# Another order for the last router unit, the z unit and the second expert tile between two phases of a fused kernel

## The reference, cut to what matters

```python
xread, sread = attention both ways between x [4,8,512,64] and state [4,8,32,64]
x = concat([xread, sread], axis=2)  -> 2176 tokens of 512      # 4 x (512 + 32)
h = x @ w_in                                                  # 512 -> 2048
x = (h * tanh(softplus(h))) @ w_out                           # 2048 -> 512
logits = cosine(x, expert_emb) / tau                          # 8 experts
e = argmax(logits); gate = softmax(logits)[e]
out = gate * (relu(x @ w1[e]) @ w2[e])                        # 512 -> 1024 -> 512
```

## Time and profile before

| what | us |
|---|---|
| median of three runs (lowest, highest) | 701.31 (697.56, 705.27) |
| the profiled execution | 701.31 |
| its span, first to last instruction | 699.5 |
| PE busy in it | 657.1 |
| DVE busy, ACT busy, POOL busy | 442.5, 385.9, 50.8 |

### The profile page before, as it was taken

How to read it: one execution, slowest core, us unless ns; L and a number is a source line. 1 busy time by engine, 2 the same in 40 slices (tenths; PEclk the granted TensorE clock), 3 DMA queues, 4 the chain that set the end, 5 groups by cost and what they waited for, 6 DMA issues and landing times.

```text
span 699.5 us, 12384 instructions
## 1 busy us (share of the span) xinstructions
PE 657.1 (94%) x4142; PEld 513.4 (73%) x4143; DVE 442.5 (63%) x687; ACT 385.9 (55%) x501; POOL 50.8 (7%) x75
## 2 busy tenths in 40 slices
PE   7889979999989999899999999889999999999995
PEld 5667657687767787676578877678888888888883
DVE  6899889979548699685677658462722452262261
ACT  2789678785547887477787453252622442261250
POOL 1000000000200002000000103001001010010101
PEclk9999999999989999999999999999999999999998
DMA  9713453000814000344000531472621360153140
GB/s 264 218 32 107 151 166 121 0 2 2 269 45 135 37 2 31 95 137 154 9 1 8 219 106 77 162 261 76 220 82 45 109 211 30 45 197 134 45 150 5
DMA packets 35350, 72.72 MB, mean 104 GB/s; under 512 B 5699, under 2 KB 5699, under 8 KB 35312
## 3 DMA queue, kind: packets, MB, share of 16 engines
q1 hardware_dynamic: 27728, 56.93, 25.3%
q0 software_dynamic: 3040, 9.13, 3.3%
q10 hardware_dynamic: 4544, 6.14, 2.9%
HBM read 60.92 MB, written 12.16 MB: 104 GB/s over the span
## 4 chain that ended last, share of the span: by engine, by line
PE 64%; DVE 16%; ACT 10%; issue 5%; DMA 4%; SPq 0%; ACTq 0%; POOL 0%; DVEq 0%; POOLq 0%
PE PS L708 16%; PE PS L736 16%; PE PS L613 11%; PE PS L569 7%; DVE ww L1384 3%; PE PS L717 3%; PE PS L524 3%; DMA raw<-in_w 2%; PE PS L478 2%; ACT ww L981 2%; DVE qq L1396 2%; ACT rr L977 2%; DVE qq L1379 2%; DVE gl L1402 2%; ACT rr L975 1%
## 5 line engine op out<-in xcount | busy, mean ns | idle before, releaser
L613 PE MATMUL PS<-WH,gh 128*128 128x512 f32 x256 | 103.3, 404 | 0.8 <-DVE gl L1402 0.8
L613 PE MATMUL PS<-WH,gl 128*128 128x512 f32 x256 | 101.0, 395 | 0.0
L613 PE MATMUL PS<-WL,gh 128*128 128x512 f32 x256 | 101.0, 394 | 0.0
L1067 ACT ACTIVATE hh<-PS 128x512 fp32r<-128x512 f32 x42 | 23.0, 596 | 96.4 <-PE PS L717 94.3
L736 PE MATMUL PS<-WH,hh 128*128 (+1 forms) x168 | 68.6, 409 | 3.1 <-DVE hl L1488 2.0
L1478 DVE TENSOR_TENSOR WL<-raw,WH 128x1024 f32 (+1 forms) x48 | 56.2, 1222 | 23.5 <-ACT WH L1047 23.4
L736 PE MATMUL PS<-WH,hl 128*128 (+1 forms) x168 | 66.5, 396 | 0.0
L736 PE MATMUL PS<-WL,hh 128*128 (+1 forms) x168 | 66.2, 394 | 0.0
L1379 DVE SCALAR_TENSOR_TENSOR qq<-ww,PS 128x1024 f32<-128x1024 f32 (+1 forms) x35 | 41.5, 1187 | 35.5 <-ACT ww L965 35.4
L981 ACT ACTIVATE ww<-ww,cst 128x1024 f32<-128x1024 f32 (+1 forms) x35 | 39.4, 1127 | 41.6 <-DVE ww L1384 41.6
L613 PEld LDWEIGHTS PS<-WH,gh 128*128 128x128 f32 x256 | 48.2, 188 | 18.8 <-issue 7.5
(11 more groups left out here) (252 smaller groups left out, 1281.8 us busy)
## 6 DMA issues: line engine op xcount, KB each, us to landing
raw<-in_w SPq DMA_DIRECT2D x48, 512.0 KB, 4.6
raw<-in_w_in SPq DMA_DIRECT2D x36, 512.0 KB, 4.9
yg<-by_expert ACTq DMA_DIRECT2D x22, 260.0 KB, 3.4
raw<-in_w_out SPq DMA_DIRECT2D x8, 512.0 KB, 4.6
by_expert<-junk SPq DMA_DIRECT2D x1, 2080.0 KB, 10.2
wr<-in_w_in SPq DMA_DIRECT2D x4, 512.0 KB, 9.4
x_0a<-in_x SPq DMA_DIRECT2D x8, 128.0 KB, 3.0
x_0b<-in_x SPq DMA_DIRECT2D x8, 128.0 KB, 3.6
```

Of the source, the lines that this page charges most:

```text
L613: mm = pe.matmul(PS[:, 2 + t, :], a[:, v % 2, e, t * P:t * P + P], w[:, 8 + p, e * 512:e * 512 + 512], start=(p == 0 and e == 0 and i == 0 ...
L1067: a.activation(hh[:, 4 * j:4 * j + 4, :], PS[:, 3 + j, :].rearrange("p (k m) -> p k m", k=4), ACT.Copy).then_inc(hh_rdy, 1)
```

## The change

`GT(3)` goes from behind step 31 to behind the first half of `YB(2)`, after the loop; `TY(t0)` goes ahead of the whole of `Y(31)`. The four transposed tiles of unit 3 use the banks 6, 3, 4, 6 in place of 3, 4, 5, 6: tile 0 waits for bank 6 to be free, and tile 3 for the copy of tile 0. `route_k(3)` goes ahead of `YB(3)`, `route_k("z")` ahead of `PB(t0)`, `TY(t1)` behind half of `PB(t0)`. On ACT `split_gz(3)` goes ahead of `y_hi(t0)`, `load(t1)` from ahead of `y_out(3)` to behind `relu(t0, 1)`, with a new wait for all scatters of unit 3; two squares go ahead of the two `turned(3, ...)`; `load(t2)` goes ahead of `h_hi(t1, 1)`. On DVE `lo_gz(3)` goes ahead of `y_lo(t0)` and `second_tile` behind `route_b(3)`. On POOL `scatter(3)` goes ahead of `root("z")`.

```diff
         def t_bank(c, t):
-            return (3, 4, 5, 6)[t] if c == 3 else 6
+            return (6, 3, 4, 6)[t] if c == 3 else 6
...
             root(3)
+            scatter(3)
             root("z")
-            scatter(3)
             scatter("z")
...
-                if c == 3 and t == 3:
+                if c == 3 and t == 0:
                     pe.wait_ge(gz_lo, 4)
+                elif c == 3 and t == 3:
+                    pe.wait_ge(rt_e, 3 * ST + 1)
...
-                if second(t):
-                    pe.wait_ge(idx_rdy, RU[3] + 1)
...
                     if p == 7:
-                        Y(v, (0,))
                         TY(t0)
-                Y(v, (1,) if v == 0 or v == B * PC - 1 else (0, 1))
+                Y(v, (1,) if v == 0 else (0, 1))
...
                     if p == 7:
-                        GT(3)
                         YB(2, (0, 1))
+            GT(3)
             for t in range(ST):
                 route_t(3, t)
             for t in range(ST):
                 route_l(3, t)
             YB(2, (2, 3))
+            route_k(3)
             YB(3)
-            route_k(3)
             PA(t0, (0,))
             route_t("z", 0)
             PA(t0, (1,))
-            t1 = (0, 1)
             TR(t0, (0,))
             route_l("z", 0)
             TR(t0, (1,))
+            route_k("z")
+            PB(t0, (0, 1, 2, 3))
+            t1 = (0, 1)
             TY(t1)
-            PB(t0, (0, 1))
-            route_k("z")
-            PB(t0, (2, 3))
             PB(t0, (4, 5))
             PA(t1)
...
                     act.wait_ge(e1_rdy, 1)
+                    act.wait_ge(scattered, 16 * 4 * ST)
...
             whi(0, 2, 0)
+            split_gz(3)
             y_hi(t0)
             whi(0, 3, 0)
+            y_out(3)
+            squares(3, (0, 1))
+            turned(3, 0)
+            turned(3, 2)
+            squares(3, (2, 3))
+            gate_exp(3)
+            y_out("z")
+            whi(0, 4, 0)
+            squares("z", (0,))
+            whi(0, 5, 0)
             t1, t2 = (0, 1), (0, 2)
-            load(t1)
-            y_out(3)
-            split_gz(3)
-            turned(3, 0)
-            squares(3, (0,))
-            turned(3, 2)
-            squares(3, (1, 2, 3))
-            whi(0, 4, 0)
-            gate_exp(3)
-            whi(0, 5, 0)
-            y_out("z")
-            squares("z", (0,))
-            whi(0, 6, 0)
             relu(t0, 0)
             turned("z", 0)
+            whi(0, 6, 0)
+            relu(t0, 1)
+            load(t1)
             whi(0, 7, 0)
-            relu(t0, 1)
             h_hi(t0, 0)
             h_hi(t0, 1)
             gate_exp("z")
...
             h_hi(t1, 0)
-            h_hi(t1, 1)
             act.wait_ge(tab_rdy, 3)
             less4 = act.value_load(etab[0:1, E_LESS4:E_LESS4 + 1], min_val=NT - 4, max_val=WT - 4)
             load(t2)
+            h_hi(t1, 1)
...
             wlo(0, 2, 0)
+            lo_gz(3)
             y_lo(t0)
             wlo(0, 3, 0)
-            second_tile()
             y_out(3)
-            lo_gz(3)
             turned(3, 1)
             turned(3, 3)
             route_a(3)
             route_b(3)
+            second_tile()
+            y_out("z")
             wlo(0, 4, 0)
             wlo(0, 5, 0)
-            y_out("z")
             wlo(0, 6, 0)
```

## The result

| | kernel before | kernel after |
|---|---|---|
| median us (lowest, highest, executions) | 700.92 (697.56, 705.27, 4) | 709.66 (705.73, 714.18, 4) |
| ratio, 95% interval | | 1.0137 [1.0101, 1.0172] |
| profiled execution, its span | 701.31, 699.5 | 706.29, 704.5 |
| mean granted clock of the profiled execution | 0.983 | 0.986 |

What follows compares the result with a forecast made beforehand. PE was taken as the bound, busy 657.1 of 699.5 us. Landing t2 4.5 us later plus 3.4 us of half clock gave +7.9: span 707.4, with 1.8 around it 709.2 us; range 703.0 to 714.0.

Steps and rivals of the forecast that it cites:

- 4.5 of waits: Between Y(31) and t2's landing: the landing comes at 449.6 in place of 445.1 us at full clock, +4.5 us.
- 3.4 of half clock: One half-clock fall at the stall ahead of route_t(3), one at that ahead of PB(t0), 1.7 us each.
- The hand-over: To unit 3's router: split_gz(3), ahead of y_out(3), waits for GT(3), so route_t(3) starts at 410.3, 3.0 us later.
- `route_k(3)` early earns: route_k(3) ahead of YB(3): 12 matmuls (2.8 us) leave the path; row numbers at 420.5, winning back all 3.9 us lost.
- The second tile: t1's DMA waits for unit 3's scatters, holding PB(t0) until 432.7; y_lo(t1) starts 6.0 us later, at 437.0.
- `load(t2)` first: load(t2) ahead of h_hi(t1,1): issued 0.95 us behind the table, landing 12.6 behind y_lo(t1) in place of 14.1, gaining 1.5.
- The clock: TensorE's half-clock falls on the new path: 3.4 us taken, from bounds of none (0) to 6.6.
- Rival (b): Half clock holds through the router, three falls in a row plus one: 4.5 + 6.6 = +11.1, 712.4 us; chance 0.19.
- Rival (a): Stalls come but the clock holds, or falls only under work off the path: +4.5, 705.8 us; chance 0.30.
- Rival (c): y_out(3), freed from load(t1), starts right behind Y(31), route_t(3) 2.3 us earlier: -3.8, 697.5 us; chance 0.05.

Runs made afterwards that it cites:

- e1: Kernel after with split_gz(3) and lo_gz(3) again behind y_out(3) and tile banks 3, 4, 5, 6: 706.68 us, ratio to before 1.0120.
- e12: Kernel after with GT(3) again ahead of the first half of YB(2): 708.47 us, ratio to before 1.0110.
- e10: e4 with TY(t1) ahead of PB(t0): 697.63 us, ratio to before 0.9963.
- e11: Kernel after with route_k(3) behind YB(3) again: 717.45 us, ratio to before 1.0249.
- e3: Kernel after with load(t1) early, behind unit 3's squares, without the wait for scatters, and second_tile ahead of route_a(3): 708.58 us, ratio to before 1.0142.
- e4: Kernel after with the edits of e1 and e3, and turned(3,0) ahead of the squares: 700.09 us, ratio to before 1.0017.
- e7: Kernel after unchanged, run again for a second profile: 709.92 us (1 execution).
- e9: Kernel after with unread matmuls cut to the stalls, 20 behind GT(3), 4 ahead of route_k("z"), 5 behind it: 704.18 us, ratio to before 1.0059.
- e5: Kernel after with unread matmuls, 36 behind GT(3), 8 ahead of route_k("z") and 10 behind it: 709.31 us, ratio to before 1.0143.
- e8: e1 unchanged, run again for a second profile: 703.93 us (1 execution).
- e6: e1 with 8 unread matmuls ahead of route_k("z") and 10 behind it: 702.51 us, ratio to before 1.0040.

## Why the prediction was right

The forecast was +7.9 us, made of 4.5 of waits and 3.4 of half clock. It was right in its mechanism, and its size is in part luck, as shown below. By its own steps, against the first profile, all times from the last matmul of `Y(31)`:

| step | forecast, full clock | measured |
|---|---|---|
| `route_t(3)` starts | 6.8 | 6.83 |
| row numbers of unit 3 done | 17.0 | 18.83 |
| DMA of t1 | 26.5 | 28.03 |
| `PB(t0)` starts | 29.2 | 30.79 |
| `y_lo(t1)` starts | 33.5 | 36.49 |
| table's last operation starts | 42.2 | 45.18 |
| t2 lands | 46.1 | 49.4 |

- **The hand-over** was right to 0.03 us in its place and in its cause, and e1, e12 and e10 show that cause: `GT(3)` sets it, and the edit that freed ACT from `load(t1)` earned nothing in the kernel after.
- **`route_k(3)` early earns** its 2.8 us, shown by e11 for the row numbers.
- **The second tile** did stand on the path, with the 2.7 us from its DMA to `PB(t0)` as forecast. Its share depends on the rest: taking the wait away from the kernel after (e3) gained 0.8 us of wait, and no time beyond the noise; from e1 (e4) it gained 6.6 us of time.
- **`load(t2)` first** earns 1.1 us on the trace, not 1.5. The mis-sized term is the time from the table to the DMA, 1.3 us for 0.95.
- **The 4.5 of waits** hold some clock. The old landing, from which the forecast counts, had a fall of its own on the path: the 18 matmuls of `YB` ahead of `route_k(3)` took 5.69 us in the chain of the kernel before, and 18 x 0.23 is 4.2. The forecast laid a new path at full clock beside this old one. With 1.5 us of half clock taken out of both, the waits are 6.0, and the clock adds 3.3 - 1.5 = 1.8 net in the profile, and 3.4 - 1.5 = 1.9 by the forecast's terms.
- **The clock** was the open term and the largest spread. From `route_t(3)` to the row numbers the profile lost 1.8 us to it, under `PB(t0)` 1.4 more; the table's last row is 3.3 over the full-clock forecast, for 3.4. That these agree is luck: I had two falls at 1.7 each; this profile has three that cost 1.1 each on average, and e7 has 17.1 us at half in a row. Rival (b), the clock held down through the router, is what e7 shows up to the counts. Of its price, 6.6 us, D shows less (9.6 over before, not 11.1): PE waited for the second part of the router and for `PB(t0)` 0.9 and 0.4 us in place of 1.0 and 1.3, with no fall behind them. Rival (a), +4.5, is what e9 approaches with the stalls filled: +4.4 us.

The executions' clocks say how much it is in the middle. The time at half clock is (1 - clock) x 2 x span: for the kernel after (0.977, median span 708.8) 32.6 us, for before (0.986, 698) 19.5. What the 13 us more cost is an estimate. If half of them is lost, it is 6.5 us. A straight line through the 32 executions of the kernel after gives 4.6 us for each 0.01 of clock, so 4.1. The 32 executions have a median of 710.5 us, 10.4 over the 700.1 of the 59 of before. e9, with nearly the clock of the kernel before, is 4.4 over it; the 6.0 of waits from above would leave 4.4 to the clock. So in the typical execution the waits are 4.4 to 6 us and the clock 4 to 6; which is larger is not shown. Against the 1.9 net of the forecast, the clock was forecast too low; the four executions of the comparison, 709.66, lay at the lower side, and that 709.2 came within 0.5 us of them is luck as well.

The Trainium skill, "TensorE: Matmul & The Clock Gate", section "HAM oscillation — how this bites in real kernels", blames idle gaps. e5 agrees: with the gaps filled no fall came. e9 agrees where the gap is and not on the rest: a fall to 0.50 follows the 8-column matmuls with the gap filled, as in the kernel before, where PE had been busy from 407.5 on.

Rival (c), faster by a free hand-over, was wrong for this change; its mechanism is what e10 carries out, worth 2.2 us and not 3.8.

What stays open is where e1 loses its time. Its first profile, 699.69, is the fastest of six executions. Their times go with the clock, from 699.69 us at 0.988 to 709.44 at 0.974: 0.014 x 2 x 705 is 20 us more at half, and half of that is the difference. But no slow one among them was profiled; e8, at 703.93, shows 1.6 us more in D and 2.6 behind it, and e6 that the stall ahead of `PB(t0)` takes part (4.2 us less when filled). The part ahead of `Y(31)`, in which the change only puts `TY(t0)` a few matmuls earlier, also differs: 401.01 us with 3.4 at half in the kernel after, 401.90 with 10.3 in e7, 403.50 with 13.6 before. So it goes with the clock only roughly, and half clock there costs less than half of its length.

## What to carry to other kernels

Before an instruction is taken out of the way of a critical one, list what then stands in front of it on each in-order engine and when the latest of those can go: here a split that waits for PE took the place of a load, and ended 3 us later. Price a stall of PE twice, once as a wait and once as the half clock under the work that follows; here the two were about equal, and unread matmuls of just the stalls' length gave 5.5 us back without any new order. See first whether the old path that you count from has half clock in it. Two causes undone one at a time may each show little: here 3.0 and 1.1 us, and 9.6 together. Compare profiles between two marks around the edit, and look at the clock of more than one execution.

## What was not expected of the hardware

- The clock stayed at half for 17 us with PE busy for 16 of them (e7), under 128x128 transpositions, 8-column matmuls and 5.9 us of mostly 128x512 matmuls. In e5 the same transpositions and 8-column matmuls ran at full clock.
- One kernel's executions spread over 8.6 us (705.7 to 714.3), and their mean granted clocks over 0.970 to 0.986, the slower ones being mostly those with the lower clock.
- A product of the identity in f32 runs as two matmuls and takes 0.23 us where a transposition of the same shape took 0.11 (four in 0.43).
